# First batch's running totals by matmuls, scores for 64 keys at a time, keys times values in the state's layout, and later loads from ACT's queue

## The reference, cut to what matters

```python
def _attn_ref(q, k, v, a_re, a_im):
    mag = np.sqrt(a_re * a_re + a_im * a_im)
    scale = np.minimum(mag, 0.999) / (mag + 1e-06)
    a_re_n, a_im_n = (a_re * scale, a_im * scale)
    for t in range(S):
        new_re = ar * S_re - ai * S_im
        new_im = ar * S_im + ai * S_re
        kv = np.einsum('bhd,bhe->bhde', k[:, :, t], v[:, :, t])
        S_re, S_im = (new_re + kv, new_im)
        y[:, :, t] = np.einsum('bhd,bhde->bhe', q[:, :, t], S_re)
```

## Time and profile before

| | |
|---|---|
| median of 3 runs | 780.65 us (779.03 to 780.88) |
| the profiled execution | 780.54 us, span 778.8 us |
| first matmul | 48.61 us |
| first scores | 55.06 us |
| MLP of batch 0 begins | about 105.5 us |
| a later batch, from scores to scores | 176.8 us, of which attention 40.7 |

### The profile page before, as it was taken

How to read it: one execution, slowest core, us unless ns; L and a number is a source line. 1 busy time by engine, 2 the same in 40 slices (tenths; PEclk the granted TensorE clock), 3 DMA queues, 4 the chain that set the end, 5 groups by cost and what they waited for, 6 DMA issues and landing times.

```text
span 778.8 us, 13125 instructions
## 1 busy us (share of the span) xinstructions
PE 710.3 (91%) x4944; PEld 683.4 (88%) x4944; DVE 503.9 (65%) x918; ACT 417.3 (54%) x913; POOL 220.8 (28%) x175
## 2 busy tenths in 40 slices
PE   0028999999999999999999999999999999999998
PEld 0027879999999979999999979999999879999998
DVE  6978858699458758597458747597448832224634
ACT  8875757665464636673464637674463621223531
POOL 0003582433430053222530053223440000113350
PEclk9998999999999999999999999999999999999999
DMA  9645540010246850010136950010136840000121
GB/s 325 201 110 144 146 176 5 1 42 1 61 120 192 218 203 21 1 42 0 61 104 193 235 203 21 0 42 1 42 103 183 227 144 37 1 1 1 42 61 61
DMA packets 42734, 73.45 MB, mean 94 GB/s; under 512 B 8784, under 2 KB 23376, under 8 KB 42672
## 3 DMA queue, kind: packets, MB, share of 16 engines
q1 hardware_dynamic: 42384, 72.23, 31.6%
q10 hardware_dynamic: 288, 0.39, 0.2%
HBM read 48.96 MB, written 4.72 MB: 69 GB/s over the span
## 4 chain that ended last, share of the span: by engine, by line
PE 83%; DVE 7%; ACT 4%; DMA 3%; issue 2%; SPq 1%; DVEq 0%; ACTq 0%
PE bank L1181 80%; DMA region<-qk 2%; PE bank L1351 1%; DVE stream L924 1%; PE bank L1262 1%; PE bank L1191 1%; PE bank L1221 1%; DMA region<-stream 1%; DVE logr L862 1%; DVE ST L954 1%; DVE qk L937 1%; DVE phasor L913 0%; DVE phasor L904 0%; SPq L333 0%; ACT scale L626 0%
## 5 line engine op out<-in xcount | busy, mean ns | idle before, releaser
L1181 PE MATMUL bank<-uT,w_sb 128*128 128x384 f32 x864 | 167.8, 342 | 0.0
L1181 PE MATMUL bank<-hT,w_sb 128*128 128x384 f32 x864 | 165.0, 337 | 0.0
L1181 PE MATMUL bank<-tok,z 128*128 128x384 f32 x864 | 158.7, 337 | 0.6 <-issue 0.2
L1181 PEld LDWEIGHTS bank<-uT,w_sb 128*128 128x128 f32 x864 | 153.1, 192 | 1.5 <-ACT uT L691 1.2
L1181 PEld LDWEIGHTS bank<-hT,w_sb 128*128 128x128 f32 x864 | 151.2, 188 | 0.3 <-DVE hT L1083 0.3
L1181 PEld LDWEIGHTS bank<-tok,z 128*128 128x128 f32 x864 | 149.3, 188 | 1.8 <-POOL tok L511 1.8
L1083 DVE SCALAR_TENSOR_TENSOR hT<-bank,hT 128x384 fp32r<-128x384 f32 x96 | 52.8, 550 | 72.0 <-ACT hT L683 71.7
L683 ACT ACTIVATE hT<-bank 128x384 fp32r<-128x384 f32 x96 | 46.5, 484 | 83.3 <-PE bank L1181 83.1
L511 POOL TENSOR_TENSOR tok<-tok_low,tok 128x768 fp32r<-128x768 f32 x20 | 38.1, 1907 | 86.8 <-ACT tok L713 86.8
L1191 PE MATMUL bank<-ident,stream 128*128 128x128 f32 x72 | 11.3, 297 | 48.6 <-DVE stream L937 48.6
L519 POOL TENSOR_TENSOR x_sb<-uT 128x384 f32<-128x384 f32 x24 | 25.1, 1074 | 102.2 <-DVE uT L1077 69.2
(11 more groups left out here) (147 smaller groups left out, 1310.7 us busy)
## 6 DMA issues: line engine op xcount, KB each, us to landing
stream<-in_qk SPq DMA_DIRECT2D x24, 384.0 KB, 3.8
tok_low<-in_w_tok SPq DMA_DIRECT2D x20, 384.0 KB, 3.5
stream<-in_a SPq DMA_DIRECT2D x19, 384.0 KB, 4.4
scale<-in_w_tok SPq DMA_DIRECT2D x16, 384.0 KB, 4.2
w_raw<-in_w SPq DMA_DIRECT2D x12, 384.0 KB, 7.6
region<-qk SPq DMA_DIRECT2D x16, 256.0 KB, 3.6
region<-stream SPq DMA_DIRECT2D x15, 256.0 KB, 3.1
stream<-in_v SPq DMA_DIRECT2D x16, 192.0 KB, 4.9
```

The costliest lines, as they stand in the source:

```text
L1181: return t.matmul(o, lhsT, rhs, start=start, stop=stop, is_transpose=turned)
```

## The change

- **Batch 0's running totals.** Its decays come with tokens on the partitions. TensorE multiplies them by constant matrices of ones and zeros (`first_sums`, `first_turns`), which gives the running sum of logarithms, measured from the chunk's middle, and the running phase in PSUM with features on the partitions. A chunk's last phase is copied (`first_carry`) and added to the next by a matmul with the identity. ACT makes the exponentials for all chunks straight from PSUM, before the arctangents, so the two table loads between go. The real part's square moves to VectorE. The scans go.
- **Scores.** Per head one matmul for the first 64 keys over 128 queries and one for the last 64 keys over the last 64 queries. Odd heads have their halves of the output partitions exchanged, and so take their v rows from a second array with its halves exchanged (`v_odd`, 96 KB more for each chunk).
- **Keys times values.** Keys stationary, v moving: the product comes out as the state lies. `turn_state` and ACT's copy go. VectorE adds it directly, and waits for the values of the same chunk before it overwrites the state.
- **Loads.** Q and K for chunks 3 on, and v likewise, are issued from ACT inside `attention` where SyncE did it. Each v load has a second DMA.
- **Weights.** The pieces of the first matrix are ordered by half; three of the splits move behind the first quotients of batch 1; the w_tc pieces load behind the first row copies.

```diff
+        SUMS = P + 2
+        first_consts = region[:, 10 * D:10 * D + 2 * SUMS + P]
+        from_mid = first_consts[:, 0:2 * SUMS].rearrange("p (k x) -> p k x", x=SUMS)
+        tri_turn = first_consts[:, 2 * SUMS:]
...
+        sums_bank = (bank[0], bank[1], bank[2])
+        turns_bank = (bank[6], bank[7], bank[5], bank[2], bank[5], bank[2])
...
+        up_pieces = (0, 1, 2, 4, 5, 6)
+        down_pieces = (3, 7, 8, 9, 10, 11)
...
+                sp.dma_start(v_odd[c % 3], v_turned[b, c * P:(c + 1) * P, :]).then_inc(s_v_in[c % 3].sem, 16)
...
-                    if c + 3 < C and (c >= 1 or b == 0):
-                        load_qk(b, c + 3)
-                    if c >= 1 and c + 2 < C:
-                        load_v(b, c + 2)
...
+                    if b == 1 and c < 3:
+                        split(EARLY + 1 + c)
...
+            def first_logs(c):
+
+                ln_m2, den, cor = logr[:, c, :], phasor[:, c, 1, :], qk[:, first_span(c)]
+                act.wait_ge(s_m2.sem, c + 1)
+                a.activation(ln_m2, ln_m2, ACT.Ln).then_inc(s_ln.sem, 1)
+                if c + 1 < C:
+                    first_square(c + 1)
+                act.wait_ge(s_ln.sem, c + 1)
+                a.activation(den, ln_m2, ACT.Exp, scale=0.5).then_inc(s_mag.sem, 1)
+                a.activation(cor, ln_m2, ACT.Exp, scale=-0.5, bias=ln_eps[:, :]).then_inc(s_eps.sem, 1)
+                act.wait_ge(s_eps.sem, c + 1)
+                a.activation(cor, cor, ACT.Ln, bias=1.0).then_inc(s_cor.sem, 1)
+                act.wait_ge(s_den.sem, c + 1)
+                a.activation(den, den, ACT.Ln).then_inc(s_lnden.sem, 1)
+                if c >= 1:
+                    first_decays(c - 1)
+                act.wait_ge(s_lnden.sem, c + 1)
+                a.activation(den, den, ACT.Exp, scale=-1.0).then_inc(s_rden.sem, 1)
+
+            def first_decays(c):
+
+                act.wait_ge(s_first_sum.sem, c + 1)
+                exponent = sums_bank[c % 3][:, 0:G * SUMS].rearrange("p (i x) -> p i x", x=SUMS)[:, :, 0:P]
+                for j, sign in enumerate((1.0, -1.0)):
+                    ins = a.activation(first_scale[:, j, first_span(c)].rearrange("p (i t) -> p i t", i=G), exponent,
+                                       ACT.Exp, scale=sign)
+                ins.then_inc(s_exp.sem, 1)
...
+                a.activation(cos, sin, ACT.Abs).then_inc(s_wrap.sem, 1)
+                act.wait_ge(s_wrap.sem, c + 1)
+                a.activation(cos, cos, ACT.Sin, scale=-SIN_TURN, bias=half_pi[:, :])
+                a.activation(sin, sin, ACT.Sin, scale=SIN_TURN).then_inc(s_phasor.sem, 1)
...
+                if c + 3 < C and (c >= 1 or b == 0):
+                    load_qk(b, c + 3)
+                if c >= 1 and c + 2 < C:
+                    load_v(b, c + 2)
-                if 1 <= c < C - 2 and (b or c >= 2):
+                if b and 1 <= c < C - 2:
                     decays(b, c + 2)
...
-                    a.activation(KV[0:112, :, :], bank[4][0:112, 0:D].rearrange("p (j d) -> p j d", j=PAIRS), ACT.Copy)\
-                        .then_inc(s_kv_sb.sem, 1)
...
+                first_logs(c)
+            first_decays(C - 1)
+            gains(0)
             nc.scalar.preload_act_table_set("trig_and_small")
             for c in range(C):
-                half_angle(0, c)
+                first_angle(c)
             for c in range(C):
                 if c == G:
-                    nc.scalar.preload_act_table_set("natural_log_exp_and_others")
-                    decays(0, 0)
-                    decays(0, 1)
-                    decays(0, 2)
                     first_rows()
-                    gains(0)
                     keys_to_sbuf(0, 0)
-                    decays(0, 3)
-                    nc.scalar.preload_act_table_set("trig_and_small")
-                if c + 1 < C:
-                    sin_cos(0, c)
...
+            def first_tangent(c):
+
+                mag, ahead = phasor[:, c, 1, :], x_sb[:, c, :]
+                dve.wait_ge(s_first_abs.sem, c + 1)
+                dve.wait_ge(s_mag.sem, c + 1)
+                d.scalar_tensor_tensor(mag, ahead, -4.0, mag, ALU.mult, ALU.add).then_inc(s_den.sem, 1)
+                if c + 1 < C:
+                    first_square_sum(c + 1)
+                dve.wait_ge(s_den.sem, c + 1)
+                d.tensor_scalar(ahead, logr[:, c, :], 0.5, math.log(0.999), ALU.mult, ALU.min).then_inc(s_lnr.sem, 1)
+                dve.wait_ge(s_rden.sem, c + 1)
+                d.tensor_tensor(mag, a_part(0, c, 1), mag, ALU.mult).then_inc(s_quot.sem, 1)
+                half_tangent(0, c)
...
+                phase, whole = phasor[:, c, 1, :], phasor[:, c, 0, :]
+                dve.wait_ge(s_phase.sem, c + 1)
+                d.tensor_scalar(whole, turns_bank[c][:, 0:D], MAGIC, MAGIC, ALU.add, ALU.subtract).then_inc(s_round.sem, 1)
+                dve.wait_ge(s_round.sem, c + 1)
+                d.tensor_tensor(phase, turns_bank[c][:, 0:D], whole, ALU.subtract).then_inc(s_frac.sem, 1)
...
-                kv = bank[2][0:2 * HD, :].rearrange("p (j e d) -> p j e d", e=2, d=64)[:, :, :, 0:HD]
-                dve.wait_ge(s_kv_t.sem, s_kv_t.at(b, c + 1))
+                kv = pairs(bank[2][0:2 * HD, 0:D].rearrange("p (h d) -> p h d", h=H))
+                dve.wait_ge(s_kv.sem, s_kv.at(b, c + 1))
...
+                if c >= 1:
+                    dve.wait_ge(s_yt.sem, s_yt.at(b, c + 1))
...
-            for c in range(C - 1):
-                if c == G + 1:
-                    queries_keys(0, 0)
-                    queries_keys(0, 1)
-                sum_turns(0, c)
-                reduce_phase(0, c)
+                    first_marks(c - 2)
+            first_marks(C - 2)
+            first_marks(C - 1)
+            first_spans()
+            scaled(0, 0)
+            split_v()
+            scaled(0, 1)
+            first_phase(0)
+            first_phase(1)
+            turned(0, 0, 0)
+            turned(0, 0, 1)
+            first_phase(2)
+            turned(0, 1, 0)
+            turned(0, 1, 1)
+            first_phase(3)
+            first_phase(4)
...
+                for i in range(G):
+                    to, at = sums_bank[c % 3][:, i * SUMS:(i + 1) * SUMS], slice(i * P, (i + 1) * P)
+                    mm(to, x_sb[:, c, at], from_mid[:, 0, :], start=i == 0, stop=False)
+                    ins = mm(to, qk[:, c * D + i * P:c * D + (i + 1) * P], from_mid[:, 1, :], start=False, stop=i == G - 1)
...
+            def first_turns(c):
+
+                pe.wait_ge(s_atan.sem, c + 1)
+                if c >= 4:
+                    pe.wait_ge(s_frac.sem, c - 1)
+                for i in range(G):
+                    to, at = turns_bank[c][:, i * P:(i + 1) * P], slice(i * P, (i + 1) * P)
+                    mm(to, phasor[:, c, 1, at], tri_turn[:, :], start=i == 0, stop=False)
+                    ins = mm(to, phasor[:, c, 0, at], tri[:, :], start=False, stop=c == 0 and i == G - 1)
+                if c >= 1:
+                    pe.wait_ge(s_carry.sem, c)
+                    for i in range(G):
+                        before = carry[:, i:i + 1].broadcast_to([P, P])
+                        ins = mm(turns_bank[c][:, i * P:(i + 1) * P], ident[:, :], before, start=False,
+                                 stop=i == G - 1)
+                ins.then_inc(s_phase.sem, 1)
 
...
-                for h in range(4):
-                    ins = mm(heads(score_bank[i][:, :])[:, h, :], rows[c % 3][0:2 * HD, 4 * i + h, 1, :],
-                             rows[c % 3][0:2 * HD, 4 * i + h, 0, :])
+                for pair in range(2):
+                    for late in range(2):
+                        for odd in range(2):
+                            h, lo, t0 = 2 * pair + odd, MID * (odd ^ late), MID * late
+                            ins = mm(heads(score_bank[i][lo:lo + MID, :])[:, h, t0:P],
+                                     rows[c % 3][0:2 * HD, 4 * i + h, 1, t0:t0 + MID],
+                                     rows[c % 3][0:2 * HD, 4 * i + h, 0, t0:P])
...
-                    pe.wait_ge(s_kv_sb.sem, s_kv_sb.at(b, c))
+                    pe.wait_ge(s_sum.sem, s_sum.at(b, c))
                 elif b:
-                    pe.wait_ge(s_out.sem, s_out.at(b - 1, KD + 1))
+                    pe.wait_ge(s_out.sem, s_out.at(b - 1, KD + 2))
+                else:
+                    pe.wait_ge(s_frac.sem, C)
                 for h in range(H):
-                    lo = 64 * (h % 2)
-                    ins = mm(bank[4][lo:lo + HD, 2 * HD * (h // 2):2 * HD * (h // 2 + 1)],
-                             v_in[c % 3][:, h * HD:(h + 1) * HD], Kn[:, h, :])
+                    ins = mm(bank[2][0:2 * HD, h * HD:(h + 1) * HD], Kn[:, h, :], v_in[c % 3][:, h * HD:(h + 1) * HD])
                 ins.then_inc(s_kv.sem, 1)
-
-            def turn_state(b, c):
-                pe.wait_ge(s_kv_sb.sem, s_kv_sb.at(b, c + 1))
-                if c >= 1:
-                    pe.wait_ge(s_sum.sem, s_sum.at(b, c))
```

(10 more changed lines are left out.)

227 lines of the change are left out of this document (146 added, 81 removed).

## The result

The changed kernel takes 794.50 us (median of 4 runs, 790.03 to 800.40) where the kernel before takes 779.84 us (4 runs, 778.96 to 780.88): a ratio of 1.0193, 95% interval 1.0157 to 1.0230. It is slower by 14.7 us, against a forecast of 774.5 us and a range of 766 to 781. The profiled execution of the changed kernel is the slowest of its four, 800.40 us (span 798.7), so its trace shows 19.9 us over the profiled execution of before.

A forecast was written before the change was run, and what follows sets the result against it. TensorE, busy 91% of 778.8 us, was taken as the bound. Batch 0 at -6.9 and three later batches at -0.4 + 0.7 (+0.9 together) took 780.54 by -6.0 to 774.5 us; range 766 to 781.

The forecast's parts named there:

- ACT's queue: Later attention stages: loads issued by ACT push the exponentials behind them; +0.7 us a batch, between -0.5 and +5.5.
- Rival 3: Chunks 1 to 3 of a later batch: load issues ahead of ACT's exponentials become the path; slower, 789 us; chance 0.1.
- The clock: Batch 0's phase sums: half clock after idling, full from the third chunk; first scores -3 (half throughout) to -5.5 us (full).
- TensorE's work per chunk: Later attention stages: scores -0.3, keys times values +0.55, transposes -0.42, form switches +0.2; sum 0.0 us (-0.75 to +0.4).
- the latencies I had put at -0.4 a batch: Later attention stages: VectorE's state update no longer waits for ACT's copy and the transposes; -0.4 us a batch.
- The start: Up to batch 0's first scores: first arctangent +2.3 us, at about 32.7; first scores -4.3 us, near 50.8.
- Chunks 0 and 1 of batch 0: Batch 0's attention: chunk 2's scores start near 67.8, not 75.53; -7.7 us, with the first scores' -4.3 in it.
- The rest of batch 0: Batch 0's later chunks: dearer keys times values counts three times, +1.5 us; shorter scores and missing transposes -0.7 at its end.
- The MLP and mixer stretches: The four stretches outside attention: no matmul there is touched, so they stay unchanged.

## Why the prediction was wrong

**The step that failed is "ACT's queue".** It priced the loads by what they push in ACT's own queue, the exponentials behind them, and held it in favour of the change that "the loads leave before those row copies instead of among them". That is so of chunk 3's row copies, which are issued from 251.85 on. Of chunk 2's, still going out, it said nothing. ACT reaches the loads of chunk 1 at 246.38 us, 0.8 us behind the first of SyncE's row copies for chunk 2 (245.55) and ahead of the last (247.46). The loads leave exactly among them. That alone cost 10.8 us in the kernel before, where the term was +0.7 a batch, +5.5 at most. The push itself came out near my +0.7: chunk 3's exponentials end 3.6 us behind chunk 1's first scores, before 2.9. TensorE never saw that push, since it was already waiting for the copies.

**Rival 3** had the side (slower), the price (789) and the point from which it decides, but another mechanism and a chance of 0.1. Its 0.85 of the DMA engines was the evidence: with the engines that busy, 672 KB issued ahead of a row copy are likely to be paid by the row copy, and here they were.

**The clock** was in the sum for the start alone. That a wait of 2.5 to 3.6 us in a later stage brings 7 to 10.6 us of half clock behind it was in none of the cases: as with the earlier trace rows, where a wait of 3.63 us did the same, the rows were on the page. Of 7.0 us that batch 1's stage lost, 2.87 are the wait and 4.6 the half clock (chunk 2 took 10.69 us in place of 6.11, the 6.47 before without their wait of 0.36); all the rest of the change together gives -0.5.

**TensorE's work per chunk** held. Forecast 0.0 (-0.75 to +0.4); by the starts of the scores, where no wait is between, +0.16 and +0.21 us (chunks 0 and 1, its wait left out), +0.05, -0.24 and -0.27 (chunks 3 to 5), with the latencies I had put at -0.4 a batch. The terms: the scores' 32 passes take 1.49 us (246.10 to 247.59) for my 1.5; keys times values 1.41 for my 1.25, 88 ns a pass. The Trainium skill's rule (TensorE: Matmul & The Clock Gate, LDWEIGHTS) made 1.7 and 1.3 of them (estimates): the products fit it, a tenth over its figure; the scores are below it. That their loads, in opposite halves, overlap in part would explain this, but no run here shows it.

**The start** came out nearly as forecast: the first arctangent at 34.04 us, not 32.7 (a table load of 1.28 at 32.75 ahead of it), the first scores at 51.53 in this execution and at 48.5 to 52.3 in those of the experiments without extra matmuls, forecast 50.8. Of the 0.7 us in this execution, half is the copies' later issue (45.86 for 45.5) and half the 4.94 us from the second copy's issue to the scores: the sum took 4.6 where its own row showed 5.0. **Chunks 0 and 1 of batch 0** were over-estimated: chunk 2's scores stand at 70.49, not 67.8. I had the half clock in chunk 5's phase sums but let the chain behind them run free; with the clock kept up, chunk 1's scores come 8.4 us behind the first ones, not 12.7. The rest of batch 0 was right (+1.6 for +1.5 in the loop, -0.3 for -0.7 at its end). **The MLP and mixer stretches** did not stay, +4.6 us in this execution. Most of it is the clock again. Behind the MLP's start the granted clock is at half for some 3.6 us in all four batches, before in batches 0 and 2 only:

```profile
289.80:293.40 3.60, 3.60 (x13) 3.52 (x13) 2.86 (x5) 1.51 (x5) 3.60 (x4) 0.53 0.20 79
284.80:288.80 4.00, 3.98 (x23) 3.82 (x23) 3.44 (x6) 2.62 (x7) 3.94 (x4) 1.00 0.32 126
```

This is batch 1, after and then before. The MLP's first 27 passes take 6.56 us there instead of 5.02, and 6.04 instead of 5.04 in batch 3. In batch 0 TensorE waits 1.09 us at 140.5 for VectorE's subtraction of u's rounded part, where before it did not. These make 3.6 of the 4.6 us; why the clock falls there, and the rest, stay open.

Not settled is how much each of the four runs of the changed kernel (790 to 800 us) lost where, since only one was profiled; their mean granted clocks, 0.972 to 0.955, fall as their times rise.

## What to carry to other kernels

When a DMA is moved to another engine's queue, line up the issue times of both queues, not the order within one. In this stage, with the DMA engines 0.85 busy, a transfer paid for what was issued ahead of its last piece, whichever queue that came from. Price a new wait of TensorE with the slow stretch that may stand behind it (here 2.9 us of wait cost 7.5), and look for it wherever the sum leaves TensorE without work. Such a wait that can't be removed can be filled with matmuls whose result is dropped, if they are counted in passes and end before the wait does.
